# First two levels of a chunked decay attention as one matrix product per stream, with three planes of prepared queries

## The reference

```python
# r, k, v, w: (4, 8, 768, 48) float32; u: (8, 48)
for t in range(S):
    cur = einsum('bhd,bhe->bhde', u[None] * kt, vt)
    y[:, :, t] = einsum('bhd,bhde->bhe', rt, state + cur)
    state = wt[:, :, :, None] * state + einsum('bhd,bhe->bhde', kt, vt)
x = y.transpose(0, 2, 1, 3).reshape(3072, 384)
x = (x @ w_a * (x @ w_b)) @ w_out                 # 384 -> 1536 -> 384
h = x @ w_in2                                     # 384 -> 2048
return (maximum(h, 0) + alpha * minimum(h, 0)) @ w_out2   # 2048 -> 384
```

## Time and profile before

| | |
|---|---|
| device time, median of 3 | 1011.13 us |
| the profiled execution | 1011.27 us, its span 1009.5 us |
| TensorE busy | 988.7 us (98% of the span) |
| VectorE busy | 558.8 us (55%) |
| ScalarE busy | 288.3 us (29%) |
| GpSimd busy | 25.4 us (3%) |
| granted TensorE clock, mean | 0.998 |

### The profile page before, as it was taken

How to read it: one execution, slowest core, us unless ns; L and a number is a source line. 1 busy time by engine, 2 the same in 40 slices (tenths; PEclk the granted TensorE clock), 3 DMA queues, 4 the chain that set the end, 5 groups by cost and what they waited for, 6 DMA issues and landing times.

```text
span 1009.5 us, 27709 instructions
## 1 busy us (share of the span) xinstructions
PE 988.7 (98%) x11776; PEld 966.2 (96%) x11776; DVE 558.8 (55%) x1124; ACT 288.3 (29%) x604; POOL 25.4 (3%) x24
## 2 busy tenths in 40 slices
PE   5899999999999999999999999999999999999998
PEld 5799999999999999999999999999999999999998
DVE  7596655655756546557432437555555555555554
ACT  3435314223242241331223325222222222222212
POOL 4500000000000000000000000000000000000000
PEclk9999999999999999999999999999999999999999
DMA  6654401312113013110020414010101010101000
GB/s 162 164 141 121 115 16 35 109 30 65 54 30 92 26 34 88 54 37 3 26 60 2 140 32 126 1 48 2 47 5 43 8 40 10 36 14 34 19 6 24
DMA packets 42130, 52.96 MB, mean 52 GB/s; under 512 B 5152, under 2 KB 42016, under 8 KB 42016
## 3 DMA queue, kind: packets, MB, share of 16 engines
q1 hardware_dynamic: 40624, 51.04, 17.6%
q10 hardware_dynamic: 1392, 0.25, 0.2%
HBM read 39.48 MB, written 9.44 MB: 48 GB/s over the span
## 4 chain that ended last, share of the span: by engine, by line
PE 96%; DVE 1%; DMA 1%; issue 1%; POOL 1%; SPq 0%; ACT 0%; DVEq 0%; POOLq 0%
PE products L166 18%; PE products L167 17%; PE products L168 17%; PE acc L168 12%; PE acc L166 12%; PE acc L167 12%; PE products L694 5%; PE products L736 1%; PE products L752 1%; PE products L721 1%; PE products L671 1%; PE products L708 1%; DMA w_v<-in_w_dram 1%; POOL r_in L490 0%; DVE f_y L920 0%
## 5 line engine op out<-in xcount | busy, mean ns | idle before, releaser
L166 PE MATMUL products<-x_parts,weights_hi 128*128 128x384 f32 x576 | 200.9, 349 | 2.6 <-DMA x_parts<-f_y 2.1
L167 PE MATMUL products<-x_parts,weights_hi 128*128 128x384 f32 x576 | 194.2, 337 | 0.0
L168 PE MATMUL products<-x_parts,weights_lo 128*128 128x384 f32 x576 | 193.9, 337 | 0.0
L1238 DVE TENSOR_SCALAR leaky_low<-products,leaky_al 128x384 f32<-128x384 f32 x128 | 79.0, 617 | 169.4 <-PE products L168 169.3
L1098 DVE TENSOR_TENSOR g_sb<-a_g,products 128x384 f32<-128x384 f32 x96 | 53.2, 554 | 187.5 <-issue 123.7
L1185 ACT ACTIVATE leaky_g_hi<-leaky_g_sb 128x384 fp32r<-128x384 f32 x128 | 67.2, 525 | 295.0 <-DVE leaky_g_sb L1243 295.0
L514 ACT ACTIVATE g_hi<-g_sb 128x384 fp32r<-128x384 f32 x96 | 50.4, 524 | 253.8 <-DVE g_sb L1098 253.8
L166 PEld LDWEIGHTS products<-x_parts,weights_hi 128*128 128x128 f32 x576 | 108.1, 188 | 7.1 <-issue 2.8
L167 PEld LDWEIGHTS products<-x_parts,weights_hi 128*128 128x128 f32 x576 | 108.2, 188 | 0.0
L168 PEld LDWEIGHTS products<-x_parts,weights_lo 128*128 128x128 f32 x576 | 108.2, 188 | 0.0
L168 PE MATMUL acc<-g_hi,weights_lo 128*128 128x384 f32 x288 | 97.5, 339 | 0.0
(11 more groups left out here) (85 smaller groups left out, 1742.1 us busy)
## 6 DMA issues: line engine op xcount, KB each, us to landing
k_in<-in_k_dram SPq DMA_DIRECT2D x16, 336.0 KB, 3.8
r_in<-in_r_dram SPq DMA_DIRECT2D x16, 336.0 KB, 5.0
stage<-in_w_out_dram SPq DMA_DIRECT2D x14, 384.0 KB, 3.2
w_v<-in_v_dram SPq DMA_DIRECT2D x16, 288.0 KB, 3.4
y_dram<-x_in SPq DMA_DIRECT2D x8, 576.0 KB, 3.0
x_in<-y_dram SPq DMA_DIRECT2D x8, 576.0 KB, 4.5
out_dram<-leaky_out_sb SPq DMA_DIRECT2D x7, 576.0 KB, 3.3
stage<-in_w_dram SPq DMA_DIRECT2D x10, 336.0 KB, 3.9
```

Source lines behind the costliest of these rows:

```text
L166: pe.matmul(out, w_hi, x_hi, start=first, stop=False)
L167: pe.matmul(out, w_hi, x_lo, start=False, stop=False)
L168: return pe.matmul(out, w_lo, x_hi, start=False, stop=last)
L1238: dve.tensor_scalar(self.low[f % 2][:, :], h, 0.0, self.al[:, f:f + 1], ALU.min, ALU.mult).then_inc(self.low_ready, 1)
```

## The change

In rounds 1 to 7 the levels h = 2 and h = 4 become one product per key block and stream. Round 0 stays.

- Stationary are the keys as they are after the first scaling (`k_first`), 62 columns. Moving are three planes of 32 queries, 96 columns: plane 0 for level 2; plane 1 for level 4 and the nearer two of its four keys; plane 2 for the farther two, with the decay over the nearer two multiplied in. Phase 2's slot has stream 0, phase 3's stream 1 (`four`), 24 products each.
- `copy_fours` (ScalarE, phases 1 and 2, after g_hi): copies of 192 and 384 elements per partition into the planes. `prepare_fours` (VectorE): 192 and 384 elements, for stream 0 at the end of phase 1, for stream 1 in phase 2.
- `merge_fours` (VectorE, phases 2 and 3): three masked copies of 384 elements each per stream, in a chain, in place of `merge_level` on 768 elements twice. The mask `four_mask` is made once, in round 0.
- `step_k` for both levels now comes after a stream's product; `step_r_four` scales 192 elements for level 2 (384 before), and for level 4 it reads the plane.
- `k_scratch` and `r_leaf` become the two halves of one tile `scratch`, whose first 1152 columns hold the planes. The next round's `prepare_r` waits for phase 3 instead of phase 0.
- b's places: in a step with its own slot but none before it (phase 2) b goes to columns 128 to 511 of bank 1, beside the fours' last columns. The last chunk of stream 0's product waits until VectorE has read that b (`g_ready`).
- `four` waits for the leaf merges, the other stream's masked copies (`fours_merged`), the ScalarE copies and the VectorE instructions for its planes.

The diff, cut to what is spoken of:

```diff
+FOUR = 2
+FOUR_STEP = 104
+Q = BLOCK // 2
...
 
 def merges(duo, phase, part):
 
-    return 12 * duo + (0 if phase == 0 else 2 * phase + 2) + part + 1
+    if duo == 0:
+        return (0 if phase == 0 else 2 * phase + 2) + part + 1
+    return 8 * duo + 4 + (0 if phase == 0 else 2 * phase - 2) + part + 1
+
+
+def fours(duo, j):
+
+    return 6 * (duo - 1) + 3 * j
...
-        k_scratch, r_leaf = ring("k_scratch", 2, [P, S]), ring("r_leaf", 2, [ROWS, S])
+        scratch = ring("scratch", 2, [P, 2 * S])
+        k_scratch, r_leaf = [tile[:, 0:S] for tile in scratch], [tile[0:ROWS, S:2 * S] for tile in scratch]
...
+            def quarters(tile, first, count, at=0):
+                return view(tile, at + FOUR * first, [[4 * FOUR, S // (4 * FOUR)], [1, FOUR * count]])
+
+            def decay_of_quarter(j, quarter, count):
+                return view(f_y, S * j + F_AT[FOUR] + quarter, [[4, S // (4 * FOUR)], [0, FOUR * count]])
+
+            def four_plane(j, plane, half=0, halves=2):
+                return view(scratch[j], TT * plane + FOUR * half, [[2 * FOUR, S // (4 * FOUR)], [1, FOUR * halves]])
...
-                at = BANK * (4 if shared_bank(g) else g % 2)
+                if shared_bank(g):
+                    at = 4 * BANK
+                elif step_at(g) is None:
+                    at = BANK * (g % 2)
+                else:
+                    at = BANK + P if slot_at(g) else 0
...
-                        act.wait_ge(products_done[j], after(n - 1, 0))
+                        act.wait_ge(products_done[j], after(n - 1, 2))
...
+                def copy_fours(n, j):
+
+                    act.wait_ge(products_done[j], after(n, 0))
+                    act.wait_ge(r_stepped[j], 6 * n + 1)
+                    copy(four_plane(j, 1, 0, 1), quarters(queries_of(n, j), 2, 1))
+                    copy(view(scratch[j], 0, [[FOUR, TT // FOUR], [1, FOUR]], ROWS), halves(queries_of(n, j), FOUR, 1)).then_inc(fours_copied[j], 1)
...
-                    if phase == 6:
+                    if n > 0 and phase in (1, 2):
+                        copy_fours(n, phase - 1)
+                    elif phase == 6:
...
-                    if phase >= 3:
+                    if phase == 5 or n == 0 and phase >= 3:
                         pe.wait_ge(merged, merges(n, phase - 2, 1))
-                    elif phase == 2 or n > 1:
+                    elif phase >= 3:
+                        pe.wait_ge(fours_merged, fours(n + 1, 0))
+                    elif phase == 2:
...
+                def four(n, j, g):
+
+                    pe.wait_ge(merged, merges(n, 0, 3))
+                    pe.wait_ge(fours_merged, fours(n, j))
+                    pe.wait_ge(k_first[j], n + 1)
+                    pe.wait_ge(fours_copied[j], n)
+                    pe.wait_ge(fours_stepped[j], 2 * n)
+                    for c in range(CH):
+                        if c == CH - 1 and j == 0:
+                            pe.wait_ge(g_ready, g + 1)
+                        for hd in range(2):
+                            for par in range(2):
+                                queries = view(scratch[j], (2 * c + par) * Q, [[TT, 3], [1, Q]], D, 64 * hd)
+                                rows = BLOCK - FOUR
+                                last = pe.matmul(view(products, 2 * BANK * hd + FOUR_STEP * c, [[1, 3 * Q]], rows, BLOCK * par),
+                                                 key_blocks(k_in[j], hd, c, par, rows), queries, start=True, stop=True)
+                    last.then_inc(products_done[j], 2)
...
+                    elif n > 0 and phase in (2, 3):
+                        four(n, phase - 2, step - BEFORE_TILES)
                     elif 2 <= phase <= 6 and step != 2:
                         level(n, phase - 1)
...
-                        pe.wait_ge(merged, merges(step_at(g) // PHASES, 0, g % 2))
+                        pe.wait_ge(merged, merges(step_at(g) // PHASES, 0, 1))
...
-                    dve.wait_ge(merged, merges(n, phase - 1, 3 if phase == 1 else 1))
+                    if n > 0 and phase == 3:
+                        dve.wait_ge(fours_merged, fours(n + 1, 0))
+                    else:
+                        dve.wait_ge(merged, merges(n, phase - 1, 3 if phase == 1 else 1))
...
+                def prepare_fours(n, j):
+
+                    dve.wait_ge(products_done[j], after(n, 0))
+                    dve.wait_ge(r_stepped[j], 6 * n + 1)
+                    dve.wait_ge(f_done, f_count(n, 0, j))
+                    dve.tensor_tensor(four_plane(j, 1, 1, 1), quarters(queries_of(n, j), 3, 1), decay_of_quarter(j, 2, 1),
+                                      ALU.mult).then_inc(fours_stepped[j], 1)
+                    dve.wait_ge(fours_copied[j], n)
+                    dve.wait_ge(fours_stepped[j], 2 * n - 1)
+                    dve.tensor_tensor(four_plane(j, 2), four_plane(j, 1), decay_of_quarter(j, 1, 2), ALU.mult).then_inc(fours_stepped[j], 1)
+
+                def merge_fours(n, j):
+
+                    def merge(columns, segment, mask, plane):
+
+                        dims = [segment, Q // segment], [1, segment]
+                        dve.copy_predicated(view(a_sb, S // 2 * j + columns, [[S, 2], [BLOCK, CH], [2 * segment, Q // segment], [1, segment]], P),
+                                            view(mask[0], mask[1], [[0, 2], [0, CH], *dims], P).bitcast(I32),
+                                            view(products, Q * plane, [[2 * BANK, 2], [FOUR_STEP, CH], *dims], P)).then_inc(fours_merged, 1)
+
+                    dve.wait_ge(products_done[j], after(n, 2))
+                    dve.wait_ge(merged, merges(n, 0, 3))
+                    dve.wait_ge(four_mask_ready, 1)
+                    dve.wait_ge(fours_merged, fours(n, j))
+                    merge(FOUR, FOUR, (level_mask, 0), 0)
+                    dve.wait_ge(fours_merged, fours(n, j) + 1)
+                    merge(2 * FOUR, 2 * FOUR, (level_mask, Q), 1)
+                    dve.wait_ge(fours_merged, fours(n, j) + 2)
+                    merge(2 * FOUR, 2 * FOUR, (four_mask, 0), 2)
...
+                def step_r_four(n, j, level):
+
+                    dve.wait_ge(r_stepped[j], 6 * n + level)
+                    dve.wait_ge(f_done, f_count(n, level - 1, j))
+                    t = queries_of(n, j)
+                    if level == 1:
+                        dve.wait_ge(fours_copied[j], n)
+                        dve.tensor_tensor(quarters(t, 1, 1), quarters(t, 1, 1), decay_of_quarter(j, 0, 1), ALU.mult).then_inc(r_stepped[j], 1)
+                    else:
+                        dve.wait_ge(fours_stepped[j], 2 * n)
+                        dve.tensor_tensor(halves(t, 2 * FOUR, 1), four_plane(j, 1), decay(n, j, 2 * FOUR, 0), ALU.mult).then_inc(r_stepped[j], 1)
...
-                    if 2 <= phase <= 5:
+                    if (4 if n > 0 else 2) <= phase <= 5:
...
                         products_of_w(n, 0, 2, range(1, 7))
+                        prepare_fours(n, 0)
+                    elif phase == 2 and n > 0:
+                        merge_fours(n, 0)
+                        prepare_fours(n, 1)
+                        step_k(n, 0, 1)
+                        step_k(n, 0, 2)
+                        step_r_four(n, 0, 1)
+                    elif phase == 3 and n > 0:
+                        merge_fours(n, 1)
+                        step_k(n, 1, 1)
+                        step_k(n, 1, 2)
+                        step_r_four(n, 0, 2)
+                        step_r_four(n, 1, 1)
+                        step_r_four(n, 1, 2)
```

More of the change, by code:

```diff
@@ L50, in view @@
     row = ap.ap[0][0]
-    return bass.AP(tensor=ap.tensor, offset=row0 * row + offset, ap=[[row, rows]] + dims)
+    return bass.AP(tensor=ap.tensor, offset=ap.offset + row0 * row + offset, ap=[[row, rows]] + dims)
 def is_zero(index):
@@ L266, in front @@
         level_mask, u_in = sb("level_mask", [P, 32 * len(MASKED)]), sb("u_in", [ROWS, 2 * PAIRS])
+        four_mask = sb("four_mask", [P, Q])
         warm = sb("warm", [P, 8])
@@ L952, in merge_level, with copy_four_mask @@
                                         view(products, level_bank(phase, 0), [[BANK, 2], [32, 2 * CH], [h, 32 // h], [1, h]], P)).then_inc(merged, 2)
+                def copy_four_mask():
+                    dve.wait_ge(masks_loaded, 32)
+                    dims = [2 * FOUR, Q // (2 * FOUR)]
+                    dve.tensor_copy(view(four_mask, 0, [dims, [FOUR, 2], [1, FOUR]], P),
+                                    view(level_mask, 0, [dims, [0, 2], [1, FOUR]], P)).then_inc(four_mask_ready, 1)
@@ L1055, in attend @@
                         copy_last_level(n)
-                    elif phase == 7 and n > 0:
+                    elif phase == 7 and n == 0:
+                        copy_four_mask()
+                    elif phase == 7:
                         step_r(n, 0, 5)
```

1 line of the change is left out of this document (added).

## The result

| | before | after |
|---|---|---|
| device time, median | 1012.22 us (5 runs) | 1017.98 us (5 runs; 1016.71 to 1018.43) |
| ratio after / before | | 1.0057, 95% interval 1.0040 to 1.0075 |
| span of the profiled execution | 1009.5 us | 1015.4 us |
| TensorE busy | 988.7 us | 988.0 us |
| VectorE busy | 558.8 us | 579.7 us |

The change makes the kernel 0.6% slower. The forecast was 1015.5 us against 1011.13, a ratio of 1.0043; its range reached to 1019. The direction and the mechanisms came as forecast; two sums were too small, and one cost was not in the forecast at all.

The account below looks back on a forecast made before the run. TensorE, busy 988.7 of 1009.5 us, was taken as the bound. Round 1 (+3.5 us) and rounds 2 to 7 (+0.9) gave +4.4 on 1011.27, 1015.7, less 0.14 to the median: 1015.5 us, range 1010.0 to 1019.0.

Parts of the forecast that it names:

- The slot's price: On TensorE, a new slot of 48 records with 96 moving columns takes 1.15 us; two save 0.64 us a round.
- Rival (a): TensorE records cost their stationary columns alone: slots of 0.75 us, 4.8 us less, 1010.7 us, no change; chance 0.13.
- The new stall of a first slot: TensorE waits 0.79 us at each first slot for planes that VectorE makes behind its f_y chain.
- The first slot's end: On TensorE, the first slot of a round ends 0.45 us late.
- the g_sb of its last chunk: The first slot's last chunk waits for g_sb at no cost: g_sb over at about 390.8, chunk at 391.2.
- ScalarE's copies: Two plane copies per stream, some 0.9 us, fit ScalarE's 2.90 us idle; costed at nothing.
- The second slot and the slot after: No TensorE stall at the second slot, nor at level 8, where VectorE's slack is 0.1 to 0.4 us.
- Rounds 2 to 7: Each of these six rounds ends 0.15 us later, +0.9 us in all.
- Round 1: VectorE has no gap: first slot 2.3 us late, up_a of the fourth step 3.85 us late; taken as 3.5 us.
- the discount of 0.35: Round 1's loss lowered from 3.85 to 3.5 us because independent VectorE instructions start 0.08 us before the other ends.
- Rival (b): VectorE's work spills over in the slot after the second: 0.7 us a phase beyond the slack, 1021.3 us; chance 0.14.
- Rival (c): VectorE's additions are hidden, so each of seven rounds gains 0.64 us: 1006.6 us, faster; chance 0.13.

Follow-up runs that it names:

- e5: Changed kernel with 64 moving columns in every new product (plane 2 left out, results incomplete): 1015.03 us, second slot 0.84 us.
- e6: Changed kernel with 32 moving columns in every new product (planes 1 and 2 left out, results incomplete): 1016.95 us, second slot 0.84 us.
- e1: Changed kernel with stream 0's planes prepared right behind the first f_y instruction, the other five moved behind g_sb of phase 2: 1013.25 us, ratio 1.0012 to before.
- e4: Changed kernel with one more 384-element VectorE instruction, into unused columns, ahead of stream 0's last plane: 1020.88 us.
- e7: Changed kernel with the last masked copy of stream 1 run twice on VectorE: 1021.07 us.
- e11: Changed kernel with tile `below` 96 columns wider, so weights and g tiles lie 512 bytes from their old places: 1017.24 us, ratio 1.0051 to before.
- e2: Changed kernel with the old two levels kept in round 1 and the new products only from round 2: 1014.83 us, ratio 1.0026 to before.
- e9: Kernel before with an unused tile of `four_mask`'s size, moving the feed-forward tiles by 128 bytes per partition: 1014.91 us, ratio 1.0035 to before.
- e10: Changed kernel with old levels in round 1, stream 0's planes earlier from round 2, and tiles 512 bytes from old places: 1008.07 us, ratio 0.9965 to before.

## Why the prediction was right, and where it was off

**The slot's price: right.** 1.15 taken, 1.15 and 1.18 measured; e5 and e6 show what sets it. Rival (a) falls.

**The new stall of a first slot: right.** 0.79 forecast, 1.04 - 0.25 = 0.79 measured, in all six rounds. e1 takes it away and e4 adds to it one for one. The first slot's end, the g_sb of its last chunk and ScalarE's copies cost nothing more, as forecast.

**The second slot and the slot after: right.** No wait in either. e7 puts the slack at 0.18 us; the forecast had 0.1 to 0.4.

**Rounds 2 to 7: a little low.** The forecast had 0.15 us a round, 0.9 in all. e11, which has the change without the shift, takes 494.35 us against 493.2: 1.15. The slots account for it: 0.79 + 1.18 + 1.15 - 2.94 = 0.18 a round, 6 x 0.18 = 1.1 (e11's own first slots idle 1.09 us and not 1.04, with which it would be 1.4).

**Round 1: the right chain, mis-sized.** The first slot was forecast at 53.56 (53.35 measured), the up_a that waits for `g_sb` at 61.95 (62.15, right behind the second slot), up_a of the fourth step at 70.0 (69.80; the execution started 0.25 earlier). The working had +3.85 us, and 3.5 was taken for overlaps between independent instructions. Relative to the start, the fourth step came 23.74 - 19.84 = 3.9 us later. Some 0.2 of that is not VectorE's own sum: the granted clock had fallen to half (see the last section), and from `g_sb` to `g_sb` this execution takes 61.17 - 53.15 = 8.02 us where e4 and e11, at the full clock there, take 7.82. In e11 the fourth step comes 23.52 us behind the start, 3.7 later than before. So the discount of 0.35 was about twice too large, and the fall of the clock was not in the forecast. The rest of the round was to hold the loss; it added 0.5 us more, in two waits that before does not have:

```profile
82.12 0.19 PEld L169 LDWEIGHTS products<-x_parts,weights_hi 128*128 128x128 f32 x1 [0.24 <-issue]
...
85.46 0.19 PEld L169 LDWEIGHTS products<-x_parts,weights_hi 128*128 128x128 f32 x1 [0.22 <-ACT a_g L541]
```

The first starts 0.12 us behind the end of `g_sb` (81.45 + 0.55). The second waits for `a_g`, which stands on ScalarE behind two weight splits. Why they are there in this execution and absent in e4 stays open. Together 4.4 instead of 3.5. e2 shows that the old code in that round gives it back (61.98).

**Not foreseen: the move of other tiles.** `four_mask` adds 128 bytes per partition to the room under the weights. The forecast took everything outside the changed slots as equal. e9 has the shift without the change, e11 the change without the shift: 1.4 us of the 5.9 by the profiles, with the medians' disagreement told above (3.5 us by e9, 0.7 by e11).

The sum of the profile: 4.4 (round 1) + 1.15 (rounds 2 to 7) + 1.4 (tiles) = 6.9, less 0.25 (earlier start) and 0.74 (the pause of before in round 2, absent after) = 5.9. The forecast of 4.4 was 1.15 short in its two own terms and 1.4 in the missing one, and the last two hid 1.0 us of that. Neither was in the forecast, so to that extent its closeness was luck.

**Rival (b)** did not occur; copies in runs of 4 cost 0.58 us for 384 elements, a bit over half of 0.98, as assumed. **Rival (a)** had called 15.1 ns a record in agreement with 12.9; they are 17% apart. Without the fixed 0.18 us a record of a level of 62 columns costs (1.49 - 0.18) / 96 = 13.6 ns, and one of e6 (0.84 - 0.18) / 48 = 13.75. **Rival (c)**, a gain of 0.64 us a round, was false for this order, but e1 shows that the order alone stood against it: with the planes ahead of the chain the additions are hidden in rounds 2 to 7. e10 has 489.17 us there against 493.2, 0.67 a round. The forecast said that the instructions "stand behind the chain in an engine that works in order", and did not ask which part of the chain they need.

## What to carry to other kernels

Shorter work on the bounding engine pays only if what it now needs is ready when the old work needed it: look at what the last producer stands behind, and move it ahead of everything that it does not read. Where a helper engine has next to no idle time, as VectorE in round 1, order helps little (0.8 us in e1), and keeping the old code there can be worth more than the gain elsewhere. When a change adds or resizes a buffer, compare the mean times of untouched instructions by operand: a move of 128 bytes per partition cost 1.4 us here by the profiles, and one of 512 bytes nothing that could be measured.

## What the runs showed of the hardware

**Operand placement and matmul time.** The mean of 128x384 products differs by 3 ns (351 or 348, 335 or 338 ns) with how far their operands were moved, in opposite directions for two groups. 0 and 512 bytes gave one pattern, 128 bytes the other; what lies between, and which operand does it, was not tried.

**The clock after short waits.** After 2.57 us of idle in round 1 the granted clock of the changed kernel fell to half (the lower level, 1.2 GHz) two us later:

```profile
53.30:54.50 1.20, 1.12 (x48) 1.06 (x48) 0.61 (x2) 0.77 (x2) 0.00 (x0) 1.00 0.95 275
54.50:56.00 1.50, 1.50 (x13) 1.47 (x7) 1.47 (x3) 1.50 (x4) 0.00 (x0) 0.71 1.06 287
56.00:57.50 1.50, 1.50 (x7) 1.50 (x6) 1.36 (x4) 0.60 (x2) 0.00 (x0) 0.50 0.36 83
57.50:59.00 1.50, 1.50 (x8) 1.50 (x7) 1.41 (x4) 0.33 (x1) 0.00 (x0) 0.66 0.00 0
```

e7 idled for 2.61 us at the same place and lost the full clock too (0.50 from 56.5 to 58.0 us). e4 idled for 3.08 us there and kept it, and so did e11 and e6 after 2.62 and 2.61; they lost it later, e11 16 us on, after 1.29 us, and e6 one step on, after 1.74 us. In the changed kernel the fall cost some 0.2 us, since VectorE led there (8.02 against 7.82 us from `g_sb` to `g_sb`); in e11 it cost over one us. The Trainium skill (TensorE: Matmul & The Clock Gate, "What's actually happening") has the point of a change depend on where in a free-running measurement the work falls. That these executions differ fits it; no run here tests it. Over all fourteen traces the pattern is plain. Of the seven with the new products in round 1, six show a stretch at the lower clock in that round behind one of the new waits (e1 and e5 too, e4 not); of the seven with the old levels there, none does. So a wait that one adds can cost more than its length, and not in each execution.
